# The first channel layer as seven block products over 768 tokens, in an attention, gated-MLP and mixer kernel

## What is computed

```python
xt = x.transpose(0, 2, 1)
h = np.maximum(xt @ w_tok1, 0.0) @ w_tok2
u = x + h.transpose(0, 2, 1)
h2 = np.maximum(u @ w_ch1, 0.0) @ w_ch2      # u: 2304 tokens x 512; w_ch1: 512 x 1536; w_ch2: 1536 x 512
return (u + h2)
```

## Time and profile before

| | us |
|---|---|
| median of 3 runs | 671.56 (671.55 to 672.13) |
| the profiled execution | 672.14 |
| its span (first to last instruction) | 670.2 |
| PE busy | 657.2 (98%) |
| DVE busy | 317.8 (47%) |
| ACT busy | 228.0 (34%) |
| POOL busy | 150.0 (22%) |

### The profile page before, as it was taken

How to read it: one execution, slowest core, us unless ns; L and a number is a source line. 1 busy time by engine, 2 the same in 40 slices (tenths; PEclk the granted TensorE clock), 3 DMA queues, 4 the chain that set the end, 5 groups by cost and what they waited for, 6 DMA issues and landing times.

```text
span 670.2 us, 11369 instructions
## 1 busy us (share of the span) xinstructions
PE 657.2 (98%) x4025; PEld 609.0 (91%) x4025; DVE 317.8 (47%) x893; ACT 228.0 (34%) x642; POOL 150.0 (22%) x237
## 2 busy tenths in 40 slices
PE   6899999999999999999999999999999999999997
PEld 5799999999999999998999999999999999999996
DVE  4887887678675887747534221221221221221211
ACT  4775356334563344633356111111111111111110
POOL 3560437411234212343348200000000000000000
PEclk9999999999999999999999999999999999999999
DMA  9838164586435864436931720400300400400101
GB/s 245 208 60 156 32 180 117 116 177 129 108 103 120 175 121 107 113 87 146 291 97 67 162 86 1 142 0 1 141 0 0 141 0 0 142 0 1 48 0 48
DMA packets 169362, 64.82 MB, mean 97 GB/s; under 512 B 126304, under 2 KB 157600, under 8 KB 169312
## 3 DMA queue, kind: packets, MB, share of 16 engines
q1 hardware_dynamic: 169312, 64.17, 37.5%
HBM read 42.91 MB, written 21.23 MB: 96 GB/s over the span
## 4 chain that ended last, share of the span: by engine, by line
PE 96%; DVE 1%; DMA 1%; issue 1%; POOL 0%; ACT 0%; SPq 0%; POOLq 0%; DVEq 0%
PE ps L1158 71%; PE ps L1259 13%; PE ps L1228 5%; PE ps L1198 4%; PE ps L1322 1%; DMA prob_blocks<-att 1%; PE ps L1177 1%; DVE att L930 0%; PE ps L1208 0%; DMA att<-prob_blocks 0%; PE ps L1247 0%; DVE att L1146 0%; ACT xT L753 0%; ACT att L723 0%; SPq L575 0%
## 5 line engine op out<-in xcount | busy, mean ns | idle before, releaser
L1158 PE MATMUL ps<-arena 128*128 128x288 f32 (+3 forms) x2064 | 352.0, 324 | 0.0
L1158 PEld LDWEIGHTS ps<-arena 128*128 128x128 f32 (+1 forms) x2064 | 323.8, 186 | 18.4
L1158 PE MATMUL ps<-arena,att_r 128*128 128x512 f32 x648 | 161.1, 393 | 0.0
L1080 DVE SCALAR_TENSOR_TENSOR att_r<-ps,att_r 128x384 fp32r<-128x384 f32 x72 | 40.1, 557 | 226.2 <-ACT att_r L833 226.1
L1158 PEld LDWEIGHTS ps<-arena,att_r 128*128 128x128 f32 x648 | 120.6, 188 | 22.0
L833 ACT ACTIVATE att_r<-ps 128x384 fp32r<-128x384 f32 x72 | 35.4, 492 | 251.1 <-PE ps L1158 251.1
L1259 PE MATMUL ps<-arena 128*128 128x288 f32 (+1 forms) x560 | 89.3, 316 | 0.0
L1259 PEld LDWEIGHTS ps<-arena 128*128 128x128 f32 x560 | 80.2, 188 | 3.9
L661 POOL TENSOR_SCALAR att<-att,rinv 128x128 f32<-128x128 f32 x144 | 54.4, 399 | 118.6 <-DVE rinv L941 118.5
L743 ACT ACTIVATE att<-att,nmax 128x128 f32<-128x128 f32 x144 | 55.8, 390 | 7.1 <-DVE nmax L930 6.7
L1228 PE MATMUL ps<-att 128*128 128x128 f32 x288 | 37.2, 276 | 2.1 <-DVE att L950 1.1
(11 more groups left out here) (77 smaller groups left out, 433.5 us busy)
## 6 DMA issues: line engine op xcount, KB each, us to landing
prob_blocks<-att SPq DMA_DIRECT2D x27, 256.0 KB, 2.6
att<-prob_blocks SPq DMA_DIRECT2D x108, 64.0 KB, 2.0
u_scratch<-uy SPq DMA_DIRECT2D x16, 288.0 KB, 2.7
att<-u_rows SPq DMA_DIRECT2D x18, 256.0 KB, 4.8
out_dram<-att SPq DMA_DIRECT2D x18, 256.0 KB, 2.1
att<-in_v_dram SPq DMA_DIRECT2D x16, 256.0 KB, 3.7
att<-in_k_dram SPq DMA_DIRECT2D x48, 72.0 KB, 2.5
att<-in_q_dram SPq DMA_DIRECT2D x48, 72.0 KB, 2.5
```

The lines of the kernel that those rows point to most:

```text
L1080: dve.scalar_tensor_tensor(out=h3[:, j % RING, 1, :], in0=ps[:, 6 + j % 2, 0:CK], scalar=0.0, in1=h3[:, j % RING, 0, :].bitcast(F32), op0= ...
L1158: ins = pe.matmul(dst, w[a], x[c], start=first and n == 0, stop=last and n == 2, skip_group_check=True)
```

## The change

The first channel layer takes 768 tokens at a time (two halves of 384) and two blocks of 128 hidden channels (`i` and `6 + i`), with the 512 inputs in two halves of 256. That is a product of 2 x 2 by 2 x 2 blocks. It was eight block products; now it is seven, of sums and differences of blocks, from whose results the four blocks of the result are put together. A block product is 6 matmuls of 384 columns (2 blocks of 128 inputs, 3 matmuls each). There are 3 stretches of 768 tokens with 6 pairs of blocks each, 18 steps in all (`NW`).

In step `n` TensorE makes the products P0 to P6 (`first_product`) into banks 6 and 7, some on top of what the bank holds. Between them stand the 12 units of the second layer of step `n - 1` (`second_product`), three at each of four places: P0 P1 (3) P2 (3) P3 P4 (3) P5 (3) P6. The four halves of the hidden blocks are finished so: ACT copies the contents of bank 6 out after P0, P2 and P4 (`copy_part`), DVE adds one of these copies to bank 7 after P1, P3 and P6 (`add_part`), and the fourth stands in bank 6 after P5. Then follow the high part on ACT (`hidden_high`) and the low part on DVE (`hidden_low`); for three of the four both now read SBUF.

The inputs need work of their own. Each step loads its two column blocks of `w_ch1` and its two row blocks of `w_ch2` anew (`load_weights`, three DMAs and 512 KB, and `load_second`, one DMA and 512 KB). DVE makes four sums of 256 columns (`weight_sums`), ACT the high part of all seven (1792 columns) and POOL the low part. The two blocks of `w_ch2` take ACT and POOL 1024 columns each (`second_high`, `second_low`). For each further stretch DVE makes four sums of 768 columns in its steps 1 and 2 (`data_sum`), ACT and POOL split seven blocks of 768 columns in steps 2 to 5 (`data_high`, `data_low`). After a stretch DVE adds `u` to six tiles in the stretch's following step (`add_rest`), and SP stores them and loads three of the six tiles of rows between the stores.

The loops are written out. The tables for the part before were written anew for all engines; their entries for attention, MLP and token mixing are the same in number, in other places. In the last table `H0`, `H1` and `wb` are gone, and `P0` to `P6`, `xe`, `ae`, `we`, `pc`, `he` (ACT), `as`, `xs`, `cs`, `dh` (DVE), `xo`, `ao`, `wo` (POOL) have come.

```diff
@@ tables (two of the 20 segments)
-        "t2 t3 a1 t4 a2 a3 a4 H0 b00 b10 b20 b30 b01 b11 b21 b31 H1").split()
+        "t2 t3 a1 t4 a2 a3 a4 P0 P1 b00 b10 b20 b30 b01 b11 b21 b31 P2 P3 P4 P5 P6").split()
...
+        SLOT_A, SLOT_X, SLOT_BANK = (0, 1, 4, 5, 3, 6, 2), (0, 1, 4, 5, 3, 2, 6), (0, 1, 0, 1, 0, 0, 1)
+        OPENS = (True, True, False, True, False, False, False)
+        AFTER_SLOT = (0, 3, 3, 0, 3, 3, 0)
...
@@ sync
+            for n in range(1, NW + 1):
+                if n + 1 < NW:
+                    sp.wait_ge(first_done, 7 * n)
+                    load_weights(n + 1)
+                if n < NW:
+                    if n >= 2:
+                        sp.wait_ge(second_done, 12 * (n - 1))
+                    load_second(n)
+                if n == 1:
+                    sp.wait_ge(*unit_full(("acc_a", B - 1, KT - 1)))
+                if n in (1, NI):
+                    sp.wait_ge(xc_sum, 4 * (n // NI + 1))
+                    for x in range(4):
+                        load_data(n // NI + 1, x)
+                if n % NI == 4:
+                    for t in range(3):
+                        load_rest(n // NI * 6 + t)
+                if n % NI == 0:
+                    for t in range(6):
+                        store((n // NI - 1) * 6 + t)
+                        if t < 3:
+                            load_rest((n // NI - 1) * 6 + t + 3)
@@ gpsimd
+            for n in range(1, NW):
+                s, i = divmod(n, NI)
+                second_low(n)
+                if n + 1 < NW:
+                    weight_low(n + 1)
+                if s + 1 < NS:
+                    for k in ((), (), (), (0, 1), (2, 3, 4), (5, 6))[i]:
+                        data_low(s + 1, k)
@@ scalar
+            for n in range(1, NW):
+                s, i = divmod(n, NI)
+                copy_part(n, 0)
+                hidden_high(n, 0)
+                second_high(n)
+                copy_part(n, 1)
+                if n + 1 < NW:
+                    weight_high(n + 1)
+                copy_part(n, 2)
+                hidden_high(n, 1)
+                hidden_high(n, 2)
...
+                hidden_high(n, 3)
@@ vector
+                if n < NW:
+                    add_part(n, 0)
+                    if n + 1 < NW:
+                        weight_sums(n + 1)
+                    hidden_low(n, 0)
+                if s + 1 < NS and i in (1, 2):
+                    data_sum(s + 1, 2 * i - 2)
+                    data_sum(s + 1, 2 * i - 1)
+                if i == 0:
+                    add_rest(r)
+                if n < NW:
+                    add_part(n, 1)
...
@@ tensor
+                if k == 0:
+                    pe.wait_ge(a_lo, n + 1)
...
+                        pe.wait_ge(h_lo, 4 * (n - 1) + 3)
+                if k == 1 and n > 0:
+                    pe.wait_ge(total_done, 3 * (n - 1) + 3)
+                if k in (2, 4, 5):
+                    pe.wait_ge(part_copied, 3 * n + (1, None, 2, 3)[k - 2])
+                if k in (3, 6):
+                    pe.wait_ge(total_done, 3 * n + (1 if k == 3 else 2))
```

More of the change, by code:

```diff
@@ new lines, in bass_attention_gmlp_mixer_kernel @@
+        OAT = WAT + 8 * DM
+        osb = [front[:, OAT + i * DM:OAT + (i + 1) * DM] for i in range(3)] + [att[:, 14 * XC:14 * XC + DM]]
+        RAT = START["xhl"] - START["w_out"] + 8 * CK
+        rest = [early[:, RAT + i * DM:RAT + (i + 1) * DM] for i in range(3)]
+        assert 2 * ASLOT <= WAT and OAT + 3 * DM <= START["w_out"] and 14 * XC <= START["tok2"] - START["w_out"]
+        assert 14 * XC + DM <= size and RAT + 3 * DM <= ARENA - START["w_out"] and XC + 4 * CK <= KD * S and KC == 12 and NS == 3
@@ L622, in _, with load_rest, store @@
[L622 to L626 removed]
+            def load_rest(r):
+                at = (r // 6 * 6 + TILE_DONE[r % 6]) * P
+                if r >= 3:
+                    sp.wait_ge(o_copied, r - 2)
+                sp.dma_start(rest[r % 3], rows_dram[at:at + P, :]).then_inc(rest_in[r % 3], 16)
+            def store(r):
+                at = (r // 6 * 6 + TILE_DONE[r % 6]) * P
+                sp.wait_ge(o_copied, r + 1)
+                sp.dma_start(rows_out[at:at + P, :], osb[r % 4]).then_inc(o_stored[r % 4], 16)
@@ L650, in _ @@
             pool.memset(mhalf[:, :], -0.5).then_inc(const_set, 1)
-            for i in range(4):
-                pool.sem_inc(o_stored[i], 16)
             pool.wait_ge(const_set, NCONST)
@@ new lines, in add_part, with hidden_low @@
+            def add_part(n, x):
+                dve.wait_ge(part_copied, 3 * n + (1, 3, 2)[x])
+                apart(dve)
+                dve.wait_ge(first_done, 7 * n + (2, 4, 7)[x])
+                dve.tensor_tensor(total[x], ps[:, 7, 0:CK], part[(0, 2, 1)[x]], ALU.add).then_inc(total_done, 1)
+            def hidden_low(n, j):
+                dve.wait_ge(h_hi, 4 * n + j + 1)
+                src = ps[:, 6, 0:CK] if j == 2 else total[(0, 1, None, 2)[j]]
+                dve.scalar_tensor_tensor(out=h_at[:, j, 1], in0=src, scalar=0.0, in1=h_at[:, j, 0].bitcast(F32),
+                                         op0=ALU.max, op1=ALU.subtract).then_inc(h_lo, 1)
@@ L1124, in _ @@
                     turn_residual(b, x)
-                elif kind == "H":
-                    hidden(0, x)
+                elif kind == "xs":
+                    data_sum(0, x)
+                elif kind == "as":
+                    weight_sums(x)
+                elif kind == "cs":
+                    add_part(0, x)
+                elif kind == "dh":
+                    hidden_low(0, x)
                 elif kind[0] == "h":
@@ L1130, in _ @@
                     piece_low(kind[1:], b, x)
[L1132 to L1152 removed]
+            for n in range(1, NW + 1):
+                s, i = divmod(n, NI)
+                r = 6 * (s - 1)
+                if n < NW:
[10 more added lines that the diff above has]
+                    add_part(n, 1)
+                if i == 0:
+                    add_rest(r + 1)
+                    add_rest(r + 2)
+                if n < NW:
+                    hidden_low(n, 1)
+                    hidden_low(n, 2)
+                if i == 0:
+                    add_rest(r + 3)
+                    add_rest(r + 4)
+                if n < NW:
+                    add_part(n, 2)
+                    hidden_low(n, 3)
+                if i == 0:
+                    add_rest(r + 5)
         @block.tensor
@@ new lines, in second_product @@
+            def second_product(n, u):
+                j, tile = u // 3, UNIT_TILE[u]
+                bank = OUT_BANK[tile]
+                if u % 3 == 0:
+                    pe.wait_ge(h_lo, 4 * n + j + 1)
+                    apart(pe)
+                if u == 0:
+                    pe.wait_ge(w2_lo, n + 1)
+                    apart(pe)
+                if n == 0 and u < 6:
+                    if bank in (4, 5):
+                        pe.wait_ge(masked, BL * B)
+                    else:
+                        pe.wait_ge(*unit_free(LAST_IN[bank]))
+                elif n % NI == 0 and u < 6:
+                    pe.wait_ge(o_copied, 6 * (n // NI - 1) + TILE_DONE.index(tile) + 1)
+                c = slice(tile % 3 * P, tile % 3 * P + P)
+                ins = product(ps[:, bank, :], [h_at[:, j, s, c] for s in range(2)], [w[n % 2][:, j % 2] for w in (w2_hi_at, w2_lo_at)],
+                              n % NI == 0 and u < 6, n % NI == NI - 1 and u >= 6)
+                ins.then_inc(second_done, 1)
```

457 lines of the change are left out of this document (223 added, 234 removed), and 26 rows, old and new, of tables (ALL_SP, FIRST_DVE, LOOP_DVE).

## The result

The changed kernel takes 683.3 us (median of 4 runs, 681.8 to 685.9) against 671.55 us before: 1.018 times as long, with a 95% interval of 1.015 to 1.021. It is slower by 11.8 us where 1.1 had been worked out. The profiled execution is the longest of the four: 685.9 us with a span of 683.4, 13.2 us longer than before. That is 2.6 us more than the median, so its trace shows somewhat more lost time than a usual execution has.

A forecast was written before the change was run, and what follows sets the result against it. TensorE alone was taken to set the time. 670.2 - 19.0 + 3.0 + 6.3 + 2.0 + 4.5 + 1.9 + 2.5 = 671.4 us of span, so 672.7 us median; own range 668.9 to 680.5, wide 662 to 688.

The forecast's parts named there:

- tables before 359 us: Part before the channel layers: same matmuls in other places, taken as 0, with -1 to +3 us left open.
- step 0: No units between its products: P5 waits 0.6 us for a copy, the next P0 2.4; together 3.0 us.
- step 1: Late load of `w_ch2` delays P4 by 3.4 us; with data sums and low parts 6.3 us in all.
- steps 2 and 8: Two data sums each with timely loads: 0.2 or 1.7 us a step, taken as 1.0 each.
- step 7: Late loads behind a store plus two data sums taking turns with POOL: next P0 late, taken as 4.5 us.
- step 13: P1 0.4 us late, and loads behind the last tile's store make P4 late: 1.9 us with the 0.4.
- the end: Rows for the last tile are issued late, so the last addition ends 3.2 us after the last matmul: 2.5 us more.
- ordinary steps: Steps of 15.7 us without a stall; chains from the loads have 1.0 to 1.1 us to spare.
- the lock: DVE operations with two SBUF inputs and POOL's wait out each other's whole instruction; without it the sum would be 7 us lower.
- Rival 3: Stalls in steps 1, 7 and 13 drop the clock to 1.2 GHz for a while: 6 us, 678 us; chance 0.12.
- Rival 1: DVE and POOL don't hinder each other; only late loads and ends count: 665.3 us, faster; chance 0.28.
- Rival 2: Load of `w_ch2` lands too late in every step, 14 us over some 14 steps: 686.7 us; chance 0.2.

The follow-up runs named there:

- w2_first: The changed kernel with SP issuing the load of `w_ch2` first of a step's four, not last; 691.4 us, ratio 1.028.
- w2_early: The changed kernel with the load of `w_ch2` issued some 1 us before the step, those of `w_ch1` at its begin; 684.4 us, ratio 1.019.
- stores: The changed kernel with the last three stores of a stretch issued behind the next step's loads; 678.6 us, ratio 1.009.
- rest6: The changed kernel with six buffers for the rows to be added, not three, all loaded in the middle of a step; 679.0 us, ratio 1.013.
- best: The changed kernel with w2_early, stores, six row buffers, earlier loads for step 1, DVE work reordered, POOL's weight low part in four instructions; 661.1 us, ratio 0.984.
- best_pool: The kernel of best with POOL making the low part of the next step's weights ahead of that of `w_ch2`; 658.8 us, ratio 0.981.
- w2_first_pool: The kernel of w2_first with POOL making the low part of the next `w_ch1` blocks ahead of that of `w_ch2`; 680.7 us, ratio 1.014.

## Why the prediction was right in its sign and short in its size

The forecast was 672.7 us. The sign came out, but the forecast's own margin over 671.56 was 1.1 us, less than the 1.3 that it called the least to be told from no change; "slower" had a chance of 0.47. So that the sign is right is in part luck. The time, 683.3, lies above the forecast's own range (668.9 to 680.5) and inside the wide one (662 to 688), which took in the rivals. The kinds of stalls were the right ones; several sizes were not.

Balance of the profiled executions against the terms of the sum. A step's term is its length, from P0 to the next P0, less 15.73 us:

| term | forecast us | measured us |
|---|---|---|
| 108 matmuls fewer | -19.0 | -19.0 |
| tables before 359 us | 0 | -1.2 |
| step 0 | 3.0 | 3.1 |
| step 1 | 6.3 | 8.8 |
| steps 2 and 8 | 2.0 | 0.3 |
| steps 4, 10 and 16 | 0 | 2.4 |
| step 7 | 4.5 | 6.6 |
| step 13 | 1.9 | 6.4 |
| the end | 2.5 | 4.9 |
| sum | 1.2 | 12.3 (13.2 in the spans; 0.9 in no term) |

- **The saving** was right: P0 begins at 357.88, and ordinary steps take 15.7 to 15.8 us, forecast 15.7.
- **Step 0** was right to the gap: 0.67 and 2.15 us, forecast 0.6 and 2.4.
- **Step 1 and the landing of `w_ch2`.** This is the step of the prediction that failed first. SP issued the load at 381.99, forecast 382.25. But it landed at 387.9, 5.9 us after the issue and not 3.7. The 3.7 us of the earlier trace rows are the median of three loads that stood 1.8 us or more apart; here it is the last of a step's four, and the runs show what that costs: 3.8 us in the median where it is the first of the four (w2_first, w2_early), 4.9 where it is the last. The trace of the kernel before had such a row: from 319.51 on it issues six loads of 384 KB half a microsecond apart, and the first landed after 3.9 us, the fourth after 5.7:

```profile
att<-in_moe_w_ch_dram SPq DMA_DIRECT2D x1, 384.0 KB, 3.9
...
att<-in_moe_w_ch_dram SPq DMA_DIRECT2D x1, 384.0 KB, 5.7
```

  P4's gap was 6.2 us from start to start, not 3.4: 2.1 for the landing, and the rest since TensorE came to P4 a microsecond sooner than forecast while the load was issued when forecast. The lock was there as well (L1149 took 4.22 us instead of 0.95), but next to that gap it cost only 0.20 us at the next P0. The sum had the gap too small and the lock too large, and they partly cancelled. That four data loads of 384 KB behind it made it late isn't shown: in step 6 the same four stood behind it, and it took 4.6.
- **Ordinary steps.** I had a spare microsecond, and there was next to none: `w_ch2` in at t = 5.8 to 6.7 where 5.1 to 5.8 was forecast, with 6.8 as the limit. In steps 4, 10 and 16 it was in at 7.4 to 7.5, and P4 waited 0.5 to 0.6 us. The limit was right to 0.1 us, as step 4 shows.
- **Steps 7 and 13.** SP's loads came behind the last store as forecast, but at t = 4.7 and 4.9, not 3.65, as the rows of the last two tiles landed 4.4 to 4.9 us after their issue (forecast 3.2). The load of `w_ch2` then took 4.5 and 5.1 to land, and P1 had waited 1.6 and 1.8 us from start to start, not 0.4. Run stores shows that this order in SP's queue costs P4 its 3.2 and 2.7 us. In step 7, 2.6 of the forecast's 4.5 us had been put down to the lock on the two sums, which cost nothing there; waits for loads and the clock alone made 6.6.
- **The end** is the same row: DVE could start 5.3 us after the last rows were issued, forecast 3.2. Run rest6 gave 4.5 of the 4.9 us back.
- **The clock.** Rival 3 was not another case but came on top: 2.2 us behind the gap in step 1 and 1.7 each in steps 7 and 13, 5.6 us together. That is what a step's term has beyond its waits, from start to start. The matmuls' own spacing agrees: in step 13 from 595.4 to 598.8 they start 0.427 us apart, not 0.231, so that half of the 3.4 us is lost. It had been given 6 us and a chance of its own, a good size; it should have been in the sum, since the forecast itself had gaps of 2 to 3.4 us. In the runs best and best_pool, without the long gaps, it doesn't fall.
- **Rival 1** (no lock) is refuted by the rows of DVE and by w2_first_pool, though the lock at its own places was nearly free in the changed kernel. **Rival 2** (each step late) did not come: ordinary steps took 15.7 to 15.8 us. It was near, as the loads were in 0.1 us before the limit.
- **Two sums of the prediction** are off by little: without the lock its sum is 7.5 us lower, as in its rival 1, not 7, and rival 3's time is 678.7, not 678.

Terms that were too small: waits for loads (2.8 us in step 1, 2.4 in steps 4, 10 and 16, 5.8 in steps 7 and 13, 2.4 at the end) and the clock (5.6), 19.0 us in all. That is 7.9 more than the 11.1 missing: the lock had been charged 7.5 us and cost 0.7 (waits of P0 behind steps 1, 2 and 8), and the tables gave back 1.2. Of the scatter between runs (681.8 to 685.9) the clock is a part: the mean granted clock was 0.990 in the shortest execution and 0.986 in the longest, by an estimate 2.7 of the 4.1 us between their spans. Only one execution of each kernel is profiled, so the rest is open.

## What to carry to other kernels

When a kernel stands at one engine's limit, a saving on that engine is worth what the new waits leave of it, and they are found step by step: for each wait take what stands ahead of it in its engine's queue, and what stands ahead of that on SP. Take the landing time of a load from rows where it stands as far back in the queue as it will in the new kernel. And with DVE and POOL both at work in SBUF, the order in which POOL takes up its work decides which of DVE's operations are held up: here one swap of two lines on POOL was worth 10.7 us in one kernel, the clock included, and 2.3 in the best.
